# Keeping a batch's attention output on chip, and spreading block means with GpSimd, in a fused attention and expert kernel

## The reference, cut to what matters

```python
# attention: B, H, S, D = 2, 8, 768, 64; block = 32, window = 16, nb = 24
k_sum = k.reshape(B, H, nb, block, D).max(axis=3)
v_sum = v.reshape(B, H, nb, block, D).mean(axis=3)
scores_l = scale * q @ k^T, kept where |row - column| < window
scores_s = scale * q @ k_sum^T + log(block)
a = softmax(concat(scores_l, scores_s));  attn = a @ concat(v, v_sum)
x = attn.transpose(0, 2, 1, 3).reshape(B * S, H * D)      # 1536 tokens x 512
# experts: each token goes to its best 2 of 8 (noisy gate), w1 512x1024, relu, w2 1024x512
logits = x @ w_gate; noise_scale = softplus(x @ w_noise); top 2, weights, sum over the two
# dense layer: leaky relu(x @ w_in) @ w_out, d_ff 2048
```

## Time and profile before

| | us |
|---|---|
| median of 3 runs | 832.32 (831.25 to 832.9) |
| the profiled execution, its own time | 827.72 |
| span of the profiled execution | 826.1 |
| PE busy in the span | 761.2 (92%) |
| POOL busy | 377.3 (46%) |
| DVE, ACT busy | 272.6, 225.2 |
| mean granted TensorE clock | 0.962 of full speed |

### The profile page before, as it was taken

One profiled execution on the slowest core, in us unless ns is written; L12 is line 12 of the kernel. 1 busy time (PEld: TensorE's weight loads), 2 busy tenths in 40 slices (PEclk: granted clock), 3 DMA queues, 4 the chain that ended last, 5 costly groups with the idle time before them and its releaser, 6 DMA issues.

```text
span 826.1 us, 12434 instructions
## 1 busy us (share of the span) xinstructions
PE 761.2 (92%) x4050; PEld 634.9 (77%) x4051; DVE 272.6 (33%) x521; ACT 225.2 (27%) x406; POOL 377.3 (46%) x326
## 2 busy tenths in 40 slices
PE   5889953995999999999999999979999999999997
PEld 4778843784778888888888888868788887888885
DVE  3866556121121222122122122146343324432223
ACT  3867440111112112122121121225222222222221
POOL 5503852878787968887979780610011001000000
PEclk9999775999899999999999999999999999999999
DMA  9999961877526364435454630344011101010001
GB/s 201 195 180 249 204 222 42 277 231 252 178 89 216 102 212 139 170 114 178 127 203 127 216 105 34 115 138 142 23 33 48 51 1 51 0 51 0 0 1 52
DMA packets 88519, 102.61 MB, mean 124 GB/s; under 512 B 55032, under 2 KB 61176, under 8 KB 88120
## 3 DMA queue, kind: packets, MB, share of 16 engines
q1 hardware_dynamic: 68488, 42.40, 21.4%
q0 software_dynamic: 14768, 52.17, 19.8%
q10 hardware_dynamic: 5232, 7.64, 2.5%
HBM read 80.35 MB, written 23.68 MB: 126 GB/s over the span
## 4 chain that ended last, share of the span: by engine, by line
PE 70%; POOL 10%; issue 8%; DMA 6%; SPq 2%; DVE 2%; ACT 1%; DVEq 0%; POOLq 0%; ACTq 0%
PE p L1225 34%; PE p L1309 5%; PE p L1311 5%; PE p L1310 5%; PE p L1324 5%; PE p L1326 5%; PE p L1325 5%; POOL w_lo L511 5%; PE p L1217 3%; POOL w_hi L509 2%; DMA stage<-in_v 1%; PE p L1212 1%; POOL stage L476 1%; DMA stage<-in_moe_w 1%; DMA x_ring<-x_tokens,token_of 1%
## 5 line engine op out<-in xcount | busy, mean ns | idle before, releaser
L511 POOL TENSOR_TENSOR w_lo<-stage,w_hi 128x1024 fp32r<-128x1024 f32 x72 | 171.8, 2386 | 6.0
L1225 PE MATMUL p<-w_hi,xT_hi 128*128 x248 | 100.0, 403 | 3.2 <-DVE xT_lo L949 1.9
L1225 PE MATMUL p<-w_hi,hT_hi 128*128 x240 | 97.7, 407 | 4.9 <-POOLq L514 4.9
L589 POOL DMA_INDIRECT y_pick<-y_by_tile,slots x20 | 19.1, 955 | 172.9 <-PE p L1296 149.3
L1225 PE MATMUL p<-w_hi,xT_lo 128*128 x248 | 97.4, 393 | 0.0
L1225 PE MATMUL p<-w_lo,xT_hi 128*128 x248 | 97.2, 392 | 0.0
L1225 PE MATMUL p<-w_lo,hT_hi 128*128 x240 | 94.9, 395 | 0.0
L1225 PE MATMUL p<-w_hi,hT_lo 128*128 x240 | 94.5, 394 | 0.0
L509 POOL TENSOR_SCALAR w_hi<-stage 128x1024 fp32r<-128x1024 f32 x72 | 76.0, 1055 | 18.9 <-DMA stage<-in_moe_w 15.9
L1309 PE MATMUL p<-f_xT_hi,w_hi 128*128 (+2 forms) x200 | 77.8, 389 | 1.5 <-DVE f_xT_lo L998 1.3
L1310 PE MATMUL p<-f_xT_lo,w_hi 128*128 (+2 forms) x200 | 76.7, 384 | 0.0
(11 more groups left out here) (194 smaller groups left out, 1245.2 us busy)
## 6 DMA issues: line engine op xcount, KB each, us to landing
stage<-in_moe_w POOLq DMA_DIRECT2D x64, 512.0 KB, 4.4
y_by_tile<-y_row ACTq DMA_DIRECT2D x29, 256.0 KB
x_by_tile<-x_ring SPq DMA_DIRECT2D x28, 256.0 KB
x_row<-x_by_tile SPq DMA_DIRECT2D x28, 256.0 KB, 2.9
v_win<-in_v SPq DMA_DIRECT2D x8, 384.0 KB
x_tokens<-x_out SPq DMA_DIRECT2D x24, 128.0 KB, 3.5
out<-f_y SPq DMA_DIRECT2D x12, 256.0 KB, 2.0
stage<-in_v SPq DMA_DIRECT2D x2, 1024.0 KB, 5.7
```

Source lines behind the costliest of these rows:

```text
L511: pool.tensor_tensor(w_lo[:, par, cols], stage[:, c % STAGES, :], w_hi[:, par, cols].bitcast(F32), ALU.subtract).then_inc(lo_split, 1)
L1225: last = nc.tensor.matmul(bank, a, w, start=(c == 0 and i == 0), stop=(c == left_hi.shape[1] - 1 and i == 2))
```

## The change

x of a whole batch stays in one tile `x_out` (128 partitions, 3 groups, 2 halves, 512 columns), which now lies where the upper part of the weight buffers will be later. `normalise` writes the 128 columns of its pair into it. The stores of batch 0 are issued once, in pair 4 behind the load of k of pair 7, as three DMAs of 512 KB in rows of 2 KB; those of batch 1 are issued at the end, behind the load of the noise. `normalise` of pair 4 and later waits for the store of batch 0 of its group. The means of a pair are fetched by one DMA of 12 KB into `mean_rows`, and POOL copies them to the 12 units with one TENSOR_SCALAR of 24 x 1536 elements, for pair 1 between the second and the third batch of block means, for pairs 2 to 5 right behind them, and for pairs 6 and 7 inside the loading of expert 0, ahead of pieces 2 and 5. PE waits for it before the first `weigh` of a pair.

```diff
@@ SP
             def load_means(n):
-                s = n % 2
-                for h in range(2):
-                    rows = vsum_dram[(2 * n + h) * NB:(2 * n + h + 1) * NB, :]
-                    sp.dma_start(v_win[WK:KC, s, h, :, 0:D], rows.unsqueeze(1).to_broadcast([NB, UNITS, D])).then_inc(v_loaded[s], 16)
+                rows = vsum_dram[2 * n * NB:2 * (n + 1) * NB, :].rearrange("(h n) d -> n h d", h=2)
+                sp.dma_start(mean_rows[WK:KC, n % 2], rows).then_inc(means_loaded[n % 2], 16)
-            def store_x(n, g):
-                sp.wait_ge(x_ready, GROUPS * n + g + 1)
-                b, lane = divmod(n, H // 2)
...
-                sp.dma_start(to, x_out[:, n % 2, g]).then_inc(x_stored[n % 2][g], 16)
+            def store_x(b, g):
+                sp.wait_ge(x_ready, GROUPS * (H // 2 * (b + 1) - 1) + g + 1)
+                to = x_dram[b * S + g * GU * QB:b * S + (g + 1) * GU * QB, :].rearrange("(u r) c -> r u c", r=P)
+                sp.dma_start(to, x_out[:, g]).then_inc(x_stored[g], 16)
...
+                        if n >= 2:
+                            sp.wait_ge(means_spread, n - 1)
                         load_means(n + 1)
...
-                if n >= 1:
+                if n == H // 2:
                     for g in range(GROUPS):
-                        store_x(n - 1, g)
+                        store_x(0, g)
@@ POOL
-                    if c == KD and between:
-                        between()
+                    if between and c in between:
+                        pool.wait_ge(lo_split, e * CHUNKS + c)
+                        between[c]()
...
+            def spread_means(n):
+                s = n % 2
+                pool.wait_ge(means_loaded[s], 16 * ((n + 1) // 2))
+                if n >= 2:
+                    pool.wait_ge(weighed, GROUPS * (n - 1))
+                pool.tensor_scalar(v_win[WK:KC, s, :, :, 0:D], mean_rows[WK:KC, s].unsqueeze(2).to_broadcast([NB, 2, UNITS, D]),
+                                   1.0, 1.0, ALU.mult, ALU.mult).then_inc(means_spread, 1)
+                pool.wait_ge(means_spread, n)
+            block_means(0)
+            block_means(1)
+            spread_means(1)
+            block_means(2)
+            for n in range(2, PAIRS - 2):
+                spread_means(n)
             pool.wait_ge(k_turned, PAIRS - 1)
...
+            between = {2: lambda: spread_means(PAIRS - 2), 5: lambda: spread_means(PAIRS - 1)}
@@ DVE, normalise(c)
-                if n >= 2:
-                    dve.wait_ge(x_stored[n % 2][g], 16 * (n // 2))
-                    dve.wait_ge(gate_turned, n - 1)
+                lane = n % (H // 2)
+                if n >= H // 2:
+                    dve.wait_ge(x_stored[g], 16)
+                    dve.wait_ge(gate_turned, n - H // 2 + 1)
@@ PE, weigh(c)
-                    pe.wait_ge(v_loaded[n % 2], (80 if n % 2 else 48) + 80 * (n // 2))
+                    pe.wait_ge(v_loaded[n % 2], 48 * (n // 2 + 1))
+                    pe.wait_ge(means_spread, n)
```

More of the change, by code:

```diff
@@ L105, in build @@
             v_mean = sb("v_mean", [P, 3, D], where=room)
-            in_block = sb("in_block", [WK, 2 * NB - 2], where=room)
+            in_block = sb("in_block", [WK, 64], where=room)[:, 0:2 * NB - 2]
+            mean_rows = sb("mean_rows", [KC, 2, 2, D], where=room)
+            sb("to_last_pieces", [P, 5 * CW - 2 * S - 3 * D - 64 - 4 * D], where=room)
+            x_out = sb("x_out", [P, GROUPS, GU // 2, DM], where=room)
         w_hi = sb("w_hi", [P, 2, WCOLS], F32R)
@@ L125, in build @@
             probsT = sb("probsT", [KC, 2, GU * P], where=room)
-            x_out = sb("x_out", [P, 2, GROUPS, GU // 2, 2 * D], where=room)
         with ExitStack() as room:
@@ L190, in build @@
         weighed = sem("weighed"); eps_added = sem("eps_added"); recip_ready = sem("recip_ready"); x_ready = sem("x_ready")
-        x_complete = sem("x_complete"); x_stored = [[sem(f"x_stored{i}{g}") for g in range(GROUPS)] for i in range(2)]
+        x_complete = sem("x_complete"); x_stored = [sem(f"x_stored{g}") for g in range(GROUPS)]; means_loaded = [sem(f"means_loaded{i}") for i in range(2)]; means_spread = sem("means_spread")
         gate_turned = sem("gate_turned"); gate_xT_ready = sem("gate_xT_ready")
@@ L366, in _ @@
             for g in range(GROUPS):
-                store_x(PAIRS - 1, g)
-            for i in range(2):
-                for g in range(GROUPS):
-                    sp.wait_ge(x_stored[i][g], 16 * (PAIRS // 2))
+                store_x(B - 1, g)
+            for g in range(GROUPS):
+                sp.wait_ge(x_stored[g], 16 * B)
             sp.sem_inc(x_complete, 1)
@@ L514, in load_weights @@
                         pool.sem_inc(w1_ready if c < KD else w2_ready, 1)
-            for i in range(3):
-                block_means(i)
-            pool.wait_ge(v_mean_done, 3)
+            def spread_means(n):
[12 more added lines that the diff above has]
+                spread_means(n)
             pool.wait_ge(k_turned, PAIRS - 1)
             settled()
-            load_weights(lambda c: weight_piece(0, c), 0, 0, reused=False)
+            between = {2: lambda: spread_means(PAIRS - 2), 5: lambda: spread_means(PAIRS - 1)}
+            load_weights(lambda c: weight_piece(0, c), 0, 0, reused=False, between=between)
             pool.wait_ge(k_turned, PAIRS)
@@ L1133, in gate_turn @@
                 for j in range(first, end):
[L1134 removed]
+                    last = nc.tensor.transpose(turned[:, j * P:(j + 1) * P], x_out[:, j // 2, j % 2, m % (H // 2) * 2 * D:(m % (H // 2) + 1) * 2 * D], ident[:])
                 last.then_inc(gate_turned, 1)
```

10 lines of the change are left out of this document (5 added, 5 removed).

## The result

| | before | changed kernel |
|---|---|---|
| median of 5 runs each, same chip | 831.9 us (829.0 to 832.9) | 836.56 us (833.57 to 838.77) |
| profiled execution, its own time | 827.72 | 838.77 |
| its span and mean granted clock | 826.1, 0.962 | 837.2, 0.95 |

The ratio is 1.0068, with an interval of 1.0037 to 1.0098: the change costs 3 to 8 us. The forecast was 836, slower. The two profiled executions lie 11 us apart, more than the medians (4.7), because the one of before is faster than any of its five timed runs and the one of after is the slowest of its five.

The account below looks back on a forecast made before the run. Bound: one chain from attention's last logits, with PE stalled by DMA on SP's busy queue. Sum: -2.7 + 9.7 + 4.0 - 7.3 + 0.3 = +4.0 us, 827.72 to 831.7 profiled, 836.3 median; range 830.0 to 842.0.

Parts of the forecast that it names:

- The prediction's own first sign: First x store's landing time: under 5 us from its issue would make the forecast wrong and A right.
- A: Rival at step 12: the store of batch 0 lands by 75.5 us, so the kernel is faster, -2.3 us, 830.2; chance 0.17.
- Stalls at 44 and 56 gone, -3.99: PE before the transposes of q: fewer DMAs on SP's queue remove both waits and the slow clock, -3.99 us.
- First spreading, +1.3: PE at `weigh(3)` waits for POOL's 1.6 us spreading of pair 1, +1.3 us (0 to 2.9).
- The wait for the store, +9.7: DVE's x_out of step 12 waits 11.0 us for the batch 0 store beside the weights; PE loses 9.7.
- POOL issues its burst from 69.6: POOL after `turn_k(6)`: four weight pieces issued from 69.6 us, sharing the engines with SP's queue from about 72.
- so they cost nothing: POOL before the burst: spreadings of pairs 2 to 5 fit its 30.82 us of idle time, cost 0.
- Clock after it, +4.0: PE after the wait for the store: lower granted clock costs 4.0 us (1.5 to 5).
- stall on k gone, -7.3: PE at 84.08: k of pair 7 issued 5 us earlier removes the stall and its slow clock, -7.3 us.
- POOL as a second path, +0.3: Before the routing: POOL's constants, late through pair 6's spreading, end at 118.7 against 119.5 by PE and DVE; +0.3 us.
- rival C: Much slower: whole burst catches k and store, then later group or pair 7's spreading stalls; +8 to +10, 841; with D 0.19.
- Rival D: Stalls at 44 and 56 come from landing times, not SP's queue, so -3.99 is missing; +7, 839; with C 0.19.

Follow-up runs that it names:

- the second pair: Kernel before and changed kernel profiled and timed again, no edit: 829.4 us (ratio 0.9997) and 836.91 us (ratio 1.0063).
- x_only: Changed kernel with only its x half: x kept for a batch, means fetched by DMA as before; 835.34 us, ratio 1.0066.
- spread1_first: Changed kernel with the spreading of pair 1 ahead of the second block means; 837.56 us, ratio 1.0069.
- spread7_sooner: Changed kernel with the spreading of pair 7 ahead of piece 4 instead of piece 5 of expert 0; 830.98 us, ratio 1.0014.
- spread7_constants: Changed kernel with the spreading of pair 7 ahead of piece 4 and POOL's constants ahead of piece 6; 829.9 us, ratio 1.0004.
- burst_first: Changed kernel with the spreading of pair 5 behind the four weight fetches of expert 0, not ahead; 840.22 us, ratio 1.0114.
- all_moved: Changed kernel with spreadings of pairs 1 and 7, constants, q and k of pair 4, means and x stores issued sooner; 828.13 us, ratio 0.9967.
- next_version: all_moved with x stores interleaved with q and k in pairs 3 and 4, and pair 2's means spread between block means; 825.94 us, ratio 0.9945.
- last_version: next_version with the spreadings of pairs 6 and 7 one piece of weights sooner, ahead of pieces 1 and 3; 824.62 us, ratio 0.9933.
- x_only_held: x_only with POOL's burst of weights held until the first x store has landed; 828.75 us, ratio 0.9978.

## Why the prediction was right, and where it was not

The number came out, and in part by luck. The sum was made for the profiled execution, +4.0 us, and carried over to the median. The medians moved by 4.7, but between the profiled executions the last logits moved by 11.5 us (8.55 in the second pair). The prediction's own first sign also went against it: a store that lands under 5 us from its issue was to mean that the forecast is wrong and A, the faster case, right. It landed in 3.8 and 4.7 us, and the kernel was slower all the same, by a wait that the sum had at nothing. By its own steps:

*Stalls at 44 and 56 gone, -3.99.* Right in size; in cause for the second only. Between `weigh(3)` and `weigh(11)` the changed kernel makes good 1.7 us in the first pair of profiles and 2.3 in the second, whose before had 1.52 and 1.91 us of such waits. It isn't all of 3.99, because PE has the lower clock behind `weigh(3)` instead (0.58 from 36 to 44 us), a cost that the sum left out: from `weigh(3)` to `weigh(4)` it takes 5.22 us where it took 3.18. The stall at 44 did not go by the shorter queue: in x_only, without stores of x there, it is 2.59 us. It became the wait for the spreading, as spread1_first shows.

*First spreading, +1.3.* Size too small in the two profiles of after, and at the upper bound of 2.9. The duration was right (1.47 for 1.6); the rest is that the second block means end at 35.4 to 36.4 rather than 33.97, so PE waits 2.9 to 3.0 us. In spread7_sooner, spread7_constants and burst_first, which are the same up to there, it waits 1.83, 2.47 and 1.19, so the size goes with the execution. In before the same lateness falls on q of pair 4. Of what the two orders give, spread1_first says that it makes no difference to the time. By the Trainium skill (GPSIMD Engine Reference, section Elementwise, side-by-side cycle accounting) a tight loop takes about 1.8 cycles an element in the best case, but the same paragraph gives 1.03 for the loops that it calls bound by the read and write ports. The 1536 elements in 1.47 us are 1.15 cycles at the page's 1.2 GHz, near the second figure, so the row of L509 was the better guide.

*The wait for the store, +9.7.* Right in kind, too large in size: PE lost 5.1 and 5.9 us in the two profiles, around the lower bound (5.7), the case I called A. The step that failed is "POOL issues its burst from 69.6". I had put the spreadings of pairs 2 to 5 into POOL's 30 us of idle time "so they cost nothing", and did not ask when their means arrive. Those of pair 5 are fetched behind `weighed` >= 12, that is at 70.66, and POOL stood at the spreading, with the burst behind it, to 77.28. x_only, without spreadings, shows the wait as I had reasoned it (13.24 on PE, against bounds of 5.7 to 13.7), and burst_first, with the burst at 68.80, shows it at 9.30 in the changed kernel itself, against my 9.7.

*Clock after it, +4.0; stall on k gone, -7.3.* The second is right: `turn_k(7)` waits for nothing. From `weigh(14)` to `weigh(17)` it is 17.66 us before and 10.59 after, so 7.1 come back. The first is smaller: from `turn_probs(15)` at 81.70 to `weigh(17)` at 94.78 it is 13.08 us, and the same stretch two pairs earlier, 55.81 to 67.30, is 11.49, so the clock cost 1.6 us there, the lower end of my 1.5 to 5 (2.6 in the second profile, against the same 11.49).

*POOL as a second path, +0.3.* This is where the loss is. I followed the spreading of pair 6 to the constants and found 118.7 beside 119.5, and never put a time on the spreading of pair 7, which stands only in rival C ("under 1 us of margin by my count"). The rows were there. The spreading of pair 7 starts 13.60 us behind the end of that of pair 6, three pieces of weights later (95.43 and 109.03). In before, from the third piece to the sixth, it is 87.65 to 100.93, or 13.28:

```profile
100.93 1.03 POOL L509 TENSOR_SCALAR w_hi<-stage 128x1024 fp32r<-128x1024 f32 x1
```

From my 91.5 for pair 6 this gives an end of 106.6, and `weigh(21)` would have been due at 105.07 + 3.7 = 108.8: two microseconds in hand, which I called under one and left at that. Both sides moved against it: pair 6 was spread 3.9 us later, because the burst was late, and PE was due 2.1 us sooner, because the store was. An early burst would not have cured it: in burst_first the means of pair 6 hold POOL up instead, and `weigh(21)` waits 2.65 us. It cost 2.6 to 3.9 us of wait and behind it 5.9 and 5.2 us of clock, against the 10.75 us that the stretch takes in spread7_sooner. spread7_sooner gives 5.9 us of the time back, and all_moved, next_version and last_version, which move the stores and the means too, come out faster than before.

So with the terms as they were measured, on the first pair of profiles: +1.4 at `weigh(20)`, +4.1 of wait at `weigh(21)`, +5.9 of clock. The forecast's +4.0 was made of a wait for the store that was 4 us too large and of no wait at the end. Rival A was right about the landing, rival C about the second place; neither alone gives the time. Rival D, that the stalls come from landing times and not from SP's queue, is refuted for the one at 56, which is gone in every profile of a kernel with either half of the change; the one at 44 hung on neither, but on the block means.

What stays open: why the second block means end at 33.4 to 37.7 us from one profile to the next. The rows of v that they wait for are asked for at the start, and in no kernel here was that part changed.

## What to carry to other kernels

When an engine gets a new task with an input of its own, look up when that input arrives, and then what stands behind the task on the engine: a wait in the idle time of an engine moves the next long chain, here the loading of weights, on which PE waited 33 us further on. Whether that is bad has to be tried: here the held-back burst also spared the store of x, and the kernel without the hold (burst_first) was the slowest of all. For every wait that a change adds, write down the time of both sides, even where it looks like the least of them. And near the end of a stage a short wait costs more than its length, where the clock drops and does not come back before the hand-over.

## What the runs showed of the hardware

A small DVE instruction can take as long as the POOL instruction beside it. DVE's 128 x 96 operations from and to SBUF, 0.21 to 0.26 us, took 2.03, 2.04, 2.36 and 2.39 us beside POOL's TENSOR_TENSOR of 128 x 1024 (2.34 to 2.35), and 0.97 to 1.03 beside its TENSOR_SCALAR (1.04); in the rows of last_version and all_moved each ends 0.06 to 0.11 us after POOL's. Others don't: the 24 reductions `negmax<-scores` (L789) took 0.65 us each in the changed kernel, beside POOL or not. The Trainium skill (GPSIMD Engine Reference, section Specifications) says that POOL shares its SBUF interfaces with VectorE, with contention for DVE instructions in a two-port mode or with two SBUF inputs. By that rule some kinds are hit and others spared, which fits the rows, though none of them shows the mode of an instruction. By where the instructions end, it is not a lower rate but a wait for the end of the other's.

The half clock was given back unevenly. After the wait of 5.11 us at 81.70 the granted clock was 0.96 in the us from 85, and after the shorter one of 3.89 us at 110.60 PE, busy in all 8 us from 112 on, stayed at 0.50 for them. No run here tells why.

Stores of 512 KB in rows of 2 KB moved 0.41 MB in a us with the engines to themselves, and the first landed 3.8 us after its issue, 4.9 in x_only_held, where the burst is held back; beside the burst of weights it took 8.0 (burst_first) and 10.3 (x_only).
